# Other places for the first batch's buffers, and an earlier split of the second batch's first two heads

## The reference

```python
scores = q @ k^T / sqrt(64)                    # 8 heads of 64
scores = where(scores >= max(scores) - tau, scores, -1e9)
x = softmax(scores) @ v                        # heads side by side: 576 x 512
xk, xr = mu * x + (1 - mu) * x_prev            # two mixes with the row before
x = sigmoid(xr @ w_r) * (relu(xk @ w_k) ** 2 @ w_v)
u = x + real(fft(fft(x, axis=rows), axis=channels))
out = u + relu(layernorm(u) @ w_ch1) @ w_ch2
```

## Time and profile before

| | |
|---|---|
| median of 3 runs | 1049.83 us (1049.58 to 1049.84) |
| the profiled execution | 1050.13 us, its span 1048.1 us |
| TensorE busy | 1006.5 us, 96% of the span |
| VectorE busy | 588.1 us, 56% |
| ScalarE busy | 476.5 us, 45% |
| GpSimd busy | 375.8 us, 36% |

### The profile page before, as it was taken

How to read it: one execution, slowest core, us unless ns; L and a number is a source line. 1 busy time by engine, 2 the same in 40 slices (tenths; PEclk the granted TensorE clock), 3 DMA queues, 4 the chain that set the end, 5 groups by cost and what they waited for, 6 DMA issues and landing times.

```text
span 1048.1 us, 19181 instructions
## 1 busy us (share of the span) xinstructions
PE 1006.5 (96%) x7440; PEld 918.2 (88%) x7440; DVE 588.1 (56%) x1196; ACT 476.5 (45%) x1102; POOL 375.8 (36%) x334
## 2 busy tenths in 40 slices
PE   6898899998999998999999999999999999999998
PEld 4676799997899997999989999888888888888998
DVE  5888896578886588785576777442123214214111
ACT  4888775746775646865657543311111111111110
POOL 0445785334564434572414246422211221111000
PEclk9999999999999999999999999999999999999999
DMA  7516121033302041301113138002001000100000
GB/s 208 186 37 193 45 56 51 11 108 102 106 25 61 13 147 51 106 25 37 48 69 112 46 126 312 5 1 73 1 1 68 6 1 37 36 1 13 24 1 36
DMA packets 39994, 67.65 MB, mean 65 GB/s; under 512 B 6368, under 2 KB 22112, under 8 KB 39392
## 3 DMA queue, kind: packets, MB, share of 16 engines
q1 hardware_dynamic: 39600, 66.10, 19.6%
q10 hardware_dynamic: 304, 0.33, 0.1%
HBM read 54.01 MB, written 12.41 MB: 63 GB/s over the span
## 4 chain that ended last, share of the span: by engine, by line
PE 79%; DVE 6%; issue 3%; ACT 2%; POOL 1%; DVEq 0%; ACTq 0%; POOLq 0%
PE PB L948 21%; PE PB L949 21%; PE PB L950 21%; PE PB L1025 7%; PE PB L1001 5%; PE PB L1019 4%; DVE neg_s L1607 2%; DVE probs L1623 1%; ACT mix_v L1416 1%; DVE mix_v L1688 1%; ACT exps L1351 1%; POOL fold_l L864 1%; ACT mix_h L1431 0%; DVE xT L1681 0%; DVE pair_dif L1844 0%
## 5 line engine op out<-in xcount | busy, mean ns | idle before, releaser
L1902 DVE SCALAR_TENSOR_TENSOR h_lo<-PB,h_hi 128x464 fp32r<-128x464 f32 (+1 forms) x80 | 51.1, 638 | 256.5 <-ACT h_hi L1570 256.5
L1570 ACT ACTIVATE h_hi<-PB 128x464 fp32r<-128x464 f32 (+1 forms) x80 | 44.3, 554 | 329.9 <-PE PB L950 329.9
L1367 ACT ACTIVATE probsT<-PB 128x256 f32<-128x256 f32 (+1 forms) x288 | 102.5, 408 | 60.1 <-PE PB L1019 59.3
L1607 DVE TENSOR_SCALAR_CACHE_REDUCE neg_s<-PB,taus 128x576 f32<-128x576 f32 x132 | 106.9, 812 | 37.0 <-PE PB L1001 26.5
L950 PE MATMUL PB<-un_h,w1l 128*128 128x464 f32 (+1 forms) x320 | 118.9, 372 | 0.0
L949 PE MATMUL PB<-h_lo,w2h 128*128 128x464 f32 (+1 forms) x320 | 118.9, 371 | 0.0
L948 PE MATMUL PB<-h_hi,w2h 128*128 128x464 f32 (+1 forms) x320 | 118.8, 371 | 0.0
L950 PE MATMUL PB<-h_hi,w2l 128*128 128x464 f32 (+1 forms) x320 | 118.8, 371 | 0.0
L948 PE MATMUL PB<-un_h,w1h 128*128 128x464 f32 (+1 forms) x320 | 118.7, 371 | 0.0
L949 PE MATMUL PB<-un_l,w1h 128*128 128x464 f32 (+1 forms) x320 | 118.6, 371 | 0.0
L1623 DVE SCALAR_TENSOR_TENSOR probs<-neg_s,thresh,exps 128x576 f32<-128x576 f32 x108 | 117.5, 1088 | 0.3 <-PE PB L1019 0.3
(11 more groups left out here) (220 smaller groups left out, 2354.3 us busy)
## 6 DMA issues: line engine op xcount, KB each, us to landing
q_raw<-qT_dram SPq DMA_DIRECT2D x54, 160.0 KB, 3.1
w_raw<-w_dram SPq DMA_DIRECT2D x8, 1024.0 KB, 8.8
k_raw<-kT_dram SPq DMA_DIRECT2D x56, 144.0 KB, 3.1
u_scr<-x2T SPq DMA_DIRECT2D x4, 1152.0 KB, 5.5
cd<-cd_scr SPq DMA_DIRECT2D x4, 1032.0 KB, 5.0
v_sb<-v_dram SPq DMA_DIRECT2D x16, 256.0 KB, 3.0
u_in<-u_scr SPq DMA_DIRECT2D x4, 928.0 KB, 5.0
out_dram<-u_in SPq DMA_DIRECT2D x16, 232.0 KB, 2.1
```

Of the source, the lines that this page charges most:

```text
L1367: nc.scalar.activation(to, bank(4 + unit % 2)[:, 0:(k1 - k0) * P128].rearrange("p (a n) -> p a n", n=P128), ACT.Copy).then_inc(unit_copied, 1)
L1607: nc.vector.tensor_scalar(negated(n).rearrange("p (a n) -> p a n", a=2), scores(n), taus[:, 2:3], None, ALU.mult, ALU.min, accum_out=negma ...
L1902: nc.vector.scalar_tensor_tensor(h_lo[:, ft % 3, 0:w], bank(4 + ft % 3)[:, 0:w], 0.0, h_hi[:, ft % 3, 0:w].bitcast(F32), ALU.max, ALU.subt ...
```

## The change

Three things are done together. The first batch's buffers get other places: `neg_third` and a new pair of tiles, `q_last` and `k_last`, lie in the memory of `xT`; `probs_even` and `probs_odd` in that of `x2T`; `probs_mixed` in that of `probs`. Pair 3's raw heads are loaded to `q_last` and `k_last`, with a semaphore of their own (`qk_last_in`), so that slot 1 of `q_raw` and `k_raw` is free after pair 1. SP loads head 9 there in slot 18, behind pair 3's; head 8 is loaded in slot 27 as before. And GpSimd splits both heads in its slots 28 to 33, by the table `first_split`, with no wait for a mask or a transpose. The third buffer of negated scores is now used up to slot 35.

```diff
 def negated_of(n):
-    if n < TILES_BATCH - 4:
-        return (n + 2) % 3
-    return (2, 1, 0, 1)[n - TILES_BATCH + 4] if in_turns(n) else n % 2
+    return (n + 2) % 3 if in_turns(n) else n % 2
...
+        r = Place(at_xT)
+        neg_third = r.put("neg_third", [P128, S], F32)
+        q_last = r.put("q_last", [P128, SQ], F32)
+        k_last = r.put("k_last", [P128, S], F32)
...
         x2T = m.put("x2T", [P128, DT, S], F32)
+        r = Place(at)
+        probs_even = r.put("probs_even", [P128, 2 * S], F32)
+        probs_odd = r.put("probs_odd", [P128, 2 * S], F32)
...
+        def raw_of(pair):
+            return (q_last[:, :], k_last[:, :]) if pair == PAIRS - 1 else (q_raw[:, pair % 2, :], k_raw[:, pair % 2, :])
...
                         if pair + 1 < PAIRS:
                             load_both(pair + 1)
-                        else:
-                            load_head(2 * PAIRS, 0)
-                    if n == TILES_BATCH:
-                        sp.wait_ge(scores_ready, TILES_BATCH)
-                        load_head(2 * PAIRS + 1, 1)
+                        if pair >= 2:
+                            load_head(2 * PAIRS + 3 - pair, 3 - pair)
...
                     if step == 1:
-                        pool.wait_ge(qk_in[p], 64 * (pair - PAIRS) + 192)
-                        if n == 1:
-                            pool.wait_ge(unit_ready, 2 * TILES_BATCH)
-                        elif n > 1:
+                        pool.wait_ge(qk_in[p], 64 * (pair - PAIRS) + (128 if p else 192))
+                        if n > 1:
...
                     if step == 4:
-                        if n == 0:
-                            pool.wait_ge(probs_ready, TILES_BATCH - 3)
...
-                second_late = {2: (1, 2, 3), 3: (4,)}
+                first_split = {1: ((0, 1),), 2: ((0, 2), (0, 3)), 3: ((0, 4),), 4: ((1, 1),), 5: ((1, 2), (1, 3)), 6: ((1, 4),)}
...
-                        pe.wait_ge(qk_in[pair % 2], 64 * (pair // 2) + 64)
+                        pe.wait_ge(arrival_of(pair), 128 if pair == 2 else 64)
```

More of the change, by code:

```diff
@@ L338, in build @@
         k_raw = m.put("k_raw", [P128, 2, S], F32)
-        at_split = m.at
         split = m.put("split", [P128, 2, SQ + 2 * S], F32R)
         q_hl, k_hi, k_lo = split[:, :, 0:SQ], split[:, :, SQ:SQ + S], split[:, :, SQ + S:SQ + 2 * S]
[L345 to L349, removed]
         v_sb = m.put("v_sb", [P128, KT, 2, 2 * DH], F32)
@@ L352, in build @@
         probs = m.put("probs", [P128, 2, S + 2 * DH], F32)
-        probs_even = Place(at).put("probs_even", [P128, 2 * S], F32)
+        probs_mixed = Place(at).put("probs_mixed", [P128, S], F32)
         at = m.at
@@ L374, in build @@
         assert r.at <= m.at
+        at = m.at
         x2T = m.put("x2T", [P128, DT, S], F32)
+        r = Place(at)
+        probs_even = r.put("probs_even", [P128, 2 * S], F32)
+        probs_odd = r.put("probs_odd", [P128, 2 * S], F32)
+        assert r.at <= m.at
         at_mix = m.at
@@ L523, in beside_outputs, with arrival_of @@
             return bank(6 + (pair + 1) % 2)
+        def raw_of(pair):
+            return (q_last[:, :], k_last[:, :]) if pair == PAIRS - 1 else (q_raw[:, pair % 2, :], k_raw[:, pair % 2, :])
+        def arrival_of(pair):
+            return qk_last_in if pair == PAIRS - 1 else qk_in[pair % 2]
         def negated(n):
@@ L623, in load_both @@
                         rows = slice(DH * half, DH * half + DH)
-                        sp.dma_start(q_raw[rows, pair % 2, :], qT[(pair * 2 + half) * DH:(pair * 2 + half + 1) * DH, :]).then_inc(qk_in[pair % 2], 16)
-                        sp.dma_start(k_raw[rows, pair % 2, :], kT[(pair * 2 + half) * DH:(pair * 2 + half + 1) * DH, :]).then_inc(qk_in[pair % 2], 16)
+                        sp.dma_start(raw_of(pair)[0][rows, :], qT[(pair * 2 + half) * DH:(pair * 2 + half + 1) * DH, :]).then_inc(arrival_of(pair), 16)
+                        sp.dma_start(raw_of(pair)[1][rows, :], kT[(pair * 2 + half) * DH:(pair * 2 + half + 1) * DH, :]).then_inc(arrival_of(pair), 16)
                 def load_next_head(pair, p):
@@ L921, in _ @@
                     pair, jj = n // TILES_PAIR, n % TILES_PAIR
-                    if pair >= PAIRS:
-                        for step in (second_late if pair == PAIRS else second_head).get(jj, ()):
+                    if pair == PAIRS - 1:
+                        for p, step in first_split.get(jj, ()):
+                            split_step(PAIRS, p, step)
+                    if pair > PAIRS:
+                        for step in second_head.get(jj, ()):
                             split_step(pair, 1, step)
-                    if PAIRS <= pair + 1 < B * PAIRS:
+                    if PAIRS < pair + 1 < B * PAIRS:
                         for step in next_head.get(jj, ()):
@@ L963, in part @@
                         width = keys.stop - keys.start
-                        return nc.tensor.matmul(scores(n + h)[:, half, at:at + width], q_raw[partitions, pair % 2, rows], k_raw[partitions, pair % 2, keys],
+                        return nc.tensor.matmul(scores(n + h)[:, half, at:at + width], raw_of(pair)[0][partitions, rows], raw_of(pair)[1][partitions, keys],
                                                 start=True, stop=True)
@@ L977, in qk_mixed @@
                     for half in range(2):
-                        last = nc.tensor.matmul(scores(n)[:, half, :], q_raw[:, pair % 2, FULL * P128:SQ], k_raw[:, pair % 2, half * HALF:(half + 1) * HALF],
+                        last = nc.tensor.matmul(scores(n)[:, half, :], raw_of(pair)[0][:, FULL * P128:SQ], raw_of(pair)[1][:, half * HALF:(half + 1) * HALF],
                                                 start=True, stop=True)
```

3 lines of the change are left out of this document (2 added, 1 removed).

## The result

The changed kernel takes 1052.16 us in the median of 22 runs (1050.26 to 1054.45), the one before 1049.84 (1049.58 to 1051.38) beside it. The ratio is 1.0017 (1.8 us), with a 95% interval of 1.0011 to 1.0023: slower by 2.3 us in the medians, 1.2 to 2.4 us by the interval. Of the kernel before, one execution among 33 beside the first experiments took 2490.56 us and is left out of their ratios.

A forecast was written before the change was run, and what follows sets the result against it. TensorE was taken as the busiest engine, waiting 2.4 us for `split` before slot 40. Terms +2.1, +0.5 and −1.1 made +1.5 us, so 1051.3 us; 8-in-10 range 1048.5 to 1053.4, the forecast's own 1050.1 to 1052.5.

The forecast's parts named there:

- The addresses and the loads cost nothing: Moved buffers change addresses only, and head 9's four loads, issued in slot 18, stay hidden: cost 0.
- GpSimd busy from 70.5 to 94 or later without a pause; the stores of the tables 1 us later at no cost: GpSimd's new order fills its last-pair pause; table stores wait until about 80 to 81.5 us, costing nothing.
- Term 1: Last pair of batch one: masks and `both_last` slowed beside busy GpSimd, +2.1 us, bounds 0 and 3.6.
- the 1.5 to 2.5 us that I had named as a sign: Profile sign in the last pair: first scores on `split` start 1.5 to 2.5 us later than 89.67.
- Term 2: First slots of batch two: one or two more masks pay 0.6 us, +0.5, between 0 and +1.
- Term 3: Slot 40: the 2.37 us wait goes, VectorE gains 0.73 and about 0.35 us; −1.1, bounds −0.7 and −2.4.
- The sign that I named for it in the profile: Slot 40's row maximum follows the first scores on `split` by 1 us or more less than 12.7 us.
- The clock, about 1 us either way: TensorE's clock dip from 110 to 112 us may stay, go or recur, blurring the time about 1 us.
- the masks have slack enough: Rival, chance 0.24: last-pair masks lose only +0.3 us, first slots of batch two nothing; −0.8 us, 1049.0.
- Full blocking: Rival, chance 0.17: four operations in slots 31 to 33 each wait for a whole GpSimd operation; +3.5 us, 1053.3.
- The whole wait comes back: Rival, chance 0.08: slot 40's 2.37 us and slow masks go, no last-pair loss; −2.4 to −3 us, 1047.1.

The follow-up runs named there:

- the first experiments: places only, second late, old table and nine first; the kernel before, run beside them, had 1050.09 us (33 runs).
- places only: Changed kernel with GpSimd's order and waits as before, keeping new addresses and earlier loads; 1049.74 us, ratio 0.9998 to the kernel before.
- second profile: The changed kernel run once more, unaltered, and profiled again; 1051.76 us (1 run).
- the memsets: Kernel before plus eight GpSimd memsets, which read nothing, in its pause of the last pair; 1050.24 us, ratio 1.0001.
- second late: Changed kernel with only head 8 split early, head 9 at its old place with its old wait; 1051.68 us, ratio 1.0018 to the kernel before.
- old table: Changed kernel with both heads' splits at their old places in GpSimd's list, without the mask and transpose waits; 1051.63 us, ratio 1.0016 to the kernel before.
- placed: As nine first, but head 9's split held until slot 23's mask, the two `wvl` until slot 32's; 1049.15 us, ratio 0.999 to the kernel before.
- nine first: Changed kernel with head 9 split right behind `cs_lo`, head 8 at its old place, no mask wait; 1050.01 us, ratio 1.0002 to the kernel before.
- busy reading: Kernel before plus six GpSimd subtractions, which read SBUF, in its pause of the last pair; 1050.69 us, ratio 1.0009.

## Why the prediction was right, and where its terms were off

The direction and the mechanism held: slower, because GpSimd's reading work in the last pair blocks VectorE's masks, more than the removed wait returns. 1051.3 was predicted and 1052.16 measured, inside the forecast's own range of 1050.1 to 1052.5. How near the number came is in part luck: up to slot 40 the mechanism is worth +1.0 us where the sum had +1.5, and more time at the lower clock, which the sum left out, made up for it. Step by step:

- *The addresses and the loads cost nothing.* Right (places only).
- *GpSimd busy from 70.5 to 94 or later without a pause; the stores of the tables 1 us later at no cost.* Right: 70.38 to 95.70, the first store at 80.99 instead of 79.99.
- *Term 1, the last pair, +2.1 at the first scores on `split`.* Too large: +1.06, and outside the 1.5 to 2.5 us that I had named as a sign. What failed is where I let the delay arrive. VectorE was 2.0 us late at the row maximum of slot 35 (89.77 instead of 87.78), as supposed, but before the change TensorE began the scores that need it at 89.67 only, 1.07 us after it was done:

```profile
87.78 0.82 DVE L1607 TENSOR_SCALAR_CACHE_REDUCE neg_s<-PB,taus 128x576 f32<-128x576 f32 x1
```

In the changed kernel TensorE goes on 0.15 us after that row maximum, so 0.92 us of the 1.07 are slack, and of the 1.99 us of lateness 1.07 should arrive, as they did. That slack was in the trace and I left it out.
- *Term 2, slots 36 and 37, +0.5.* Too small: +1.1 (from 1.06 to 2.20). It is mostly the rest of the same 2 us, arriving one slot later, where TensorE was already waiting before the change; 0.2 us are new, the mask at 91.06 with 1.75 us instead of 1.53. The sum of both terms, +2.6 predicted and +2.2 measured, was nearly right.
- *Term 3, slot 40, −1.1.* Right in size: from the end of TensorE's spread to the row maximum of slot 40 it was 102.39 less 98.66, 3.73 us, and is 104.98 less 102.44, 2.54: −1.19. The spread before:

```profile
98.05 0.61 PE L1025 MATMUL PB<-ident,rowinv 128*64 128x128 f32 x8
```

The parts fit too: 0.73 us are VectorE's old idle time, and 0.38 the mixing (0.52 us instead of 0.90, with GpSimd idle in front of it instead of splitting). What comes last there is a chain behind the spread: ScalarE's mixing, for which VectorE waits 2.12 us until 104.17, then VectorE's mixing and the copy until 105.06. VectorE's mixing starts 1.73 us after the end of the spread in both kernels. TensorE then waits 1.72 us for the row maximum at 105.85. The sign that I named for it in the profile was badly chosen, though: counted from the first scores on `split`, the row maximum came 14.25 us later (12.66 in the second profile), not under 11.7, because term 2 and the clock lie between.
- *The clock, about 1 us either way, left out of the sum.* By the mechanism alone the changed kernel is +0.99 us at slot 40 (second profile), against +1.5 predicted. Of the medians' +2.3 some 1.3 us are thus not explained by slots 28 to 40. In the first profile 1.6 us of lateness arose during the 3.4 us at the lower clock from 94.9, and both profiles have 6.8 us more of it than the kernel before. The mean granted clock of each execution, which was recorded with its time, says how far that holds for the others (59 of the kernel before have it, those beside the experiments):

| mean granted clock | kernel before: median us (executions) | changed: median us (executions) |
|---|---|---|
| 0.995 | 1049.82 (39) | 1051.11 (9) |
| 0.993 | 1051.07 (18) | 1052.66 (4) |
| 0.992 | none | 1054.33 (4) |
| 0.990 | none | 1053.06 (2) |

(Five executions, two of the kernel before and three of the changed one, lie at 0.994, 0.996 and 0.997.) So at the same mean clock the changed kernel takes 1.3 to 1.6 us more, and the remaining 0.7 to 1.0 of the 2.3 us go with its meeting the lower clock more often. Why it does so stays open. Lateness isn't needed for it: of the 11 executions with the memsets, where nothing was late, eight had 0.993 (median 1050.53) and three 0.995 (1049.76, as the kernel before). And second late and old table, whose profiles have no more of the lower clock than the kernel before, have medians 1.6 and 1.5 us up that their shifts at slot 40 explain. Placed gains less in the times than at slot 40: at 0.995 its five executions have 1049.35, 0.5 us under the kernel before; where the rest goes was not followed.

Of the rivals, *the masks have slack enough* is half true and was the most instructive: masks in the first half of a pair do have it (nine first, placed), the mask, `both_last` and mask around a mixed tile don't. Nor does the mask just ahead of them, that of slot 30, have enough: at 1.66 us (busy reading) and 1.72 us (old table) it made the row maximum of slot 32 late by 0.7 us. *Full blocking* happened as described for `both_last` and the mask behind it (1.62 and 1.89 us), with GpSimd busy from 83 to 88 us as its condition had it, but not for the other two of its four masks (0.94 and 0.89 us): the row maximum of slot 35 was 2.0 us late instead of 2.4 to 3.6, and 0.92 us of that ended in TensorE's slack for one slot. *The whole wait comes back* is refuted by that chain of mixing and copy, in placed too, where nothing disturbed it: −1.13.

## What to carry to other kernels

Moving work to an idle engine is free only if that engine's operands don't block another's: before filling a pause of GpSimd with operations that read SBUF, look which VectorE instructions with two inputs in SBUF run there, and whether they come in a row with a waiting TensorE behind them. Copies within SBUF belong to the list, though they have one input (see below). A wait in the bottleneck engine's timeline is worth what the next engine's queue would give back, here 1.1 of 2.4 us, not its length. And a delay is to be followed to the point where the waiting engine asks for it: what it had to spare there comes off first.

## What the runs showed of the hardware that was not expected

A mask beside eight memsets of GpSimd took 0.81 to 0.82 us, beside six subtractions up to 1.75: writing alone did not block it. VectorE's row maxima, which read PSUM, kept their 0.8 us beside a reading GpSimd (0.82 at 88.21 in the changed kernel, with GpSimd's subtraction from 87.30 to 89.22). But a copy of 128x576 from SBUF to SBUF, with a single input, took 0.95 us at 96.75 in the kernel before, beside GpSimd's rounding from 96.17 to 97.39, and 0.45 at 101.21 with GpSimd idle. And the same kernel's two profiles had TensorE at the lower clock at different places (3.4 us from 94.9, 6.8 from 112 and 6.8 from 419 in the one; 10.2 from 105.9, 3.4 from 266 and 3.4 from 420 in the other), so that one profile of it ended 2.6 us before the other while the row maxima from slot 4 to slot 37 agreed to 0.06 us.
